# Moving the first sums of squares and the high and low parts of the gate's input in an attention and MoE kernel

## What is computed

```python
attn = softmax(mask(scale * q @ k.T)); x = attn @ v          # x: 1536 rows, 512 columns
rms = np.sqrt(np.mean(x * x, axis=-1, keepdims=True) + 1e-06)
xn = x / rms * rms_g
g = xn @ w_gate
silu = g * (1.0 / (1.0 + np.exp(-g)))
val = xn @ w_val
return (silu * val @ w_out).astype(np.float32)
```

## Time and profile before

| | before |
|---|---|
| median of 3 runs | 808.73 us (807.5 to 809.12) |
| the profiled execution | 808.62 us, span 806.8 us |
| TensorE busy | 778.0 us |
| VectorE busy | 501.6 us |
| ScalarE busy | 374.6 us |
| GpSimd busy | 317.8 us |

### The profile page before, as it was taken

How to read it: one execution, slowest core, us unless ns; L and a number is a source line. 1 busy time by engine, 2 the same in 40 slices (tenths; PEclk the granted TensorE clock), 3 DMA queues, 4 the chain that set the end, 5 groups by cost and what they waited for, 6 DMA issues and landing times.

```text
span 806.8 us, 14337 instructions
## 1 busy us (share of the span) xinstructions
PE 778.0 (96%) x4306; PEld 689.1 (85%) x4306; DVE 501.6 (62%) x979; ACT 374.6 (46%) x668; POOL 317.8 (39%) x340
## 2 busy tenths in 40 slices
PE   7899999999989999999999999999889999999995
PEld 5789888988878999999999988888778887777884
DVE  7999999999984554434343434363674556655640
ACT  5888888888983311111101234434433425553331
POOL 7877777788886363234422002211100111010110
PEclk9999999999997999999999999999999999999999
DMA  7888769656300222111210030031543476455410
GB/s 197 236 233 217 209 165 273 182 140 159 83 2 28 91 68 65 39 39 39 65 52 0 2 155 27 26 133 35 187 157 131 140 247 230 148 199 191 140 51 22
DMA packets 53717, 96.84 MB, mean 120 GB/s; under 512 B 6841, under 2 KB 21189, under 8 KB 53656
## 3 DMA queue, kind: packets, MB, share of 16 engines
q1 hardware_dynamic: 48648, 84.90, 35.7%
q10 hardware_dynamic: 2768, 4.87, 2.3%
q0 software_dynamic: 2240, 6.31, 2.0%
HBM read 58.51 MB, written 21.04 MB: 99 GB/s over the span
## 4 chain that ended last, share of the span: by engine, by line
PE 83%; DVE 8%; issue 3%; POOL 2%; ACT 2%; DMA 1%; ACTq 0%; POOLq 0%; DVEq 0%
PE ps_t L1052 13%; PE ps_s L920 12%; PE ps_t L1122 11%; PE ps_s L1102 11%; PE ps_t L920 6%; PE ps_t L872 6%; DVE pT_l L1470 3%; PE ps_o L920 3%; PE ps_p L920 3%; PE ps_s L859 2%; PE ps_s L858 2%; DVE negmax L1452 2%; PE ps_s L1113 2%; PE ps_o L887 1%; PE ps_o L889 1%
## 5 line engine op out<-in xcount | busy, mean ns | idle before, releaser
L693 POOL TENSOR_SCALAR probs<-probs,rden,alone 128x768 f32<-128x768 f32 x96 | 94.5, 997 | 35.1 <-DVE rden L1464 34.9
L1470 DVE TENSOR_TENSOR pT_l<-ps_t,pT_h 128x384 fp32r<-128x384 f32 x192 | 97.7, 549 | 16.1 <-ACT pT_h L1212 15.0
L801 POOL DMA_INDIRECT out_dram<-rows_out,rows_in x16 | 23.0, 1440 | 194.0 <-ACT rows_out L1367 185.1
L920 PE MATMUL ps_s<-xn,w_h 128*128 128x384 f32 x384 | 98.8, 338 | 0.2 <-POOL w_l L713 0.2
L1212 ACT ACTIVATE pT_h<-ps_t 128x384 fp32r<-128x384 f32 x192 | 85.4, 491 | 25.6 <-PE ps_t L872 24.5
L1202 ACT ACTIVATE probs<-ps_s,negmax 128x768 f32<-128x768 f32 x96 | 87.0, 907 | 19.2 <-DVE negmax L1452 18.7
L872 PE MATMUL ps_t<-ident,probs 128*128 128x128 f32 x576 | 88.5, 284 | 5.7 <-DVE pT_l L1470 2.7
L1630 DVE TENSOR_TENSOR expert_w<-piece,expert_w 128x2048 f32 (+1 forms) x32 | 72.1, 2288 | 32.3 <-ACT expert_w L1335 26.7
L1452 DVE TENSOR_REDUCE negmax<-ps_s 128x1 f32<-128x770 f32 x96 | 90.8, 947 | 1.7 <-PE ps_s L859 1.1
L872 PEld LDWEIGHTS ps_t<-ident,probs 128*128 128x128 f32 x576 | 63.5, 142 | 25.8 <-DVE pT_l L1470 10.3
L1122 PE MATMUL ps_t<-expert_w,hidT_h 128*128 (+1 forms) x256 | 82.2, 402 | 2.3 <-DVE hidT_l L1785 1.4
(11 more groups left out here) (248 smaller groups left out, 1722.2 us busy)
## 6 DMA issues: line engine op xcount, KB each, us to landing
piece<-in_moe_w_dram SPq DMA_DIRECT2D x32, 1024.0 KB, 6.3
routed<-filler SPq DMA_DIRECT2D x52, 257.0 KB, 4.6
k_a<-qk_h SPq DMA_DIRECT2D x28, 192.0 KB
rows_in<-routed ACTq DMA_DIRECT2D x17, 257.0 KB, 2.7
rawv<-in_v_dram SPq DMA_DIRECT2D x8, 384.0 KB, 6.0
w_raw<-in_moe_w_gate_dram SPq DMA_DIRECT2D x12, 256.0 KB, 3.0
w_raw<-in_moe_w_val_dram SPq DMA_DIRECT2D x12, 256.0 KB, 3.4
wo_raw<-in_moe_w_out_dram SPq DMA_DIRECT2D x12, 256.0 KB, 2.6
```

What stands on the lines that cost most here:

```text
L693: nc.gpsimd.tensor_scalar(pr, pr, rden[:, j:j + 1], alone[:, j:j + 1], ALU.mult, ALU.add).then_inc(norm_done, 1)
L920: mm = nc.tensor.matmul(unit_banks[tg][w][:, 0:G], a_[par][:, w, c, :], xn_at(tg, part, c), start=(n == 0), stop=(n == 3 * C - 1))
L1470: nc.vector.tensor_tensor(pT_l[u % 4][:], ps_t[kt % 2][:, 0:G], pT_h[u % 4][:].bitcast(F32), ALU.subtract).then_inc(low_ready, 1)
```

## The change

In the last pair, ScalarE's high parts of batch 0 are made in eight pieces of 384 columns (steps 1, 2, 4, 5, 7, 8, 10, 11) and not in four of 768 (steps 1, 2, 4, 5). TensorE's sum_squares(0) and (1) move from step 1 of the tail to the ends of steps 7 and 10 of the last pair; the second goes to bank ps_o. VectorE copies each result to rms at the end of its own step 7 or 10 (sums_to_rms), counted by sums_out, for which TensorE waits before it uses the bank again (step 9 of the last pair, step 0 of the tail). The root moves from step 1 to step 0 of the tail and the high parts of batch 1 from steps 0, 2, 3 to 1, 2, 3; invert, turn_rinv and rows_of_factors move from step 2 to step 1. VectorE's low parts for the gate go as 2, 2, 1, 1, 2 in steps 0 to 4 and four after the steps (before: 2, 2, 0, 4, 2 and two). For tg 2 and 3 VectorE adds last_square into the partial sum (add_last), so TensorE has three products for each and not six. In high_of the lines behind the new return are not reached. The lines with the names of the two new semaphores, last_added and sums_out, are left out:

```diff
@@ -226,8 +226,7 @@
         POOL_LOWS = [(0, c) for c in range(C)]
-        DVE_LOWS = ([(1, c) for c in range(C)] + [(2, c) for c in range(C - 1)] + [(3, c) for c in range(C - 1)]
-                    + [(2, C - 1), (3, C - 1)])
+        DVE_LOWS = ([(1, c) for c in range(C)] + [(tg, c) for tg in (2, 3) for c in range(C)])
         addr[0] = x2_offset
@@ -383,18 +382,23 @@
         value_banks = (ps_o, ps_p)
-        sum_places = tuple(ps_p[:, HT * tg:HT * (tg + 1)] for tg in range(TG))
+        sum_places = tuple((ps_p, ps_o, ps_p, ps_p)[tg][:, HT * tg:HT * (tg + 1)] for tg in range(TG))
         SQUARES_01 = 12
+        LATE_LOWS = {0: slice(0, 2), 1: slice(2, 4), 2: slice(4, 5), 3: slice(5, 6), 4: slice(6, 8)}
         EARLY = {0: 2, 1: 6, 2: 2, 3: 2, 4: 2, 5: 2}
         def high_of(tg, c):
+
+            if tg < TG // 2:
+                return C * tg + c + 1
+            return 2 * C + c + (1 if c < C - 1 else tg - 1)
             if tg < TG // 2:
 ...
             return C + c + 1 if c < C - 1 else C + c + tg - 1
-        XNH_DONE = 2 * C + 1
+        XNH_DONE = 3 * C + 1
         first_proj_banks = (ps_o, ps_p, ps_t[0], ps_t[1])
@@ -898,8 +902,7 @@
                     pe.wait_ge(factors_row, 1)
-                    pe.wait_ge(last_squared, tg - TG // 2 + 1)
-                    parts.append(last_square[tg - TG // 2])
+                    pe.wait_ge(last_added, tg - TG // 2 + 1)
                 for t in range(HT):
@@ -949,10 +952,10 @@
                         scores(P, par, j)
-                    if not s and j == 1:
-                        pe.wait_ge(x_done, 4 * LAST_PAIR + 2)
-                        sum_squares(0)
-                        sum_squares(1)
+                    if s and not ahead and j == 9:
+                        pe.wait_ge(sums_out, 1)
+                    if not s and j == 0:
+                        pe.wait_ge(sums_out, 2)
                     if not s and j == 3:
@@ -961,9 +964,13 @@
                         values(Pv, par if j >= LAG + 1 else 1 - par, g, jj)
+                    if s and not ahead and j in (7, 10):
+                        pe.wait_ge(x_done, 4 * LAST_PAIR + (j - 7) // 3)
+                        sum_squares((j - 7) // 3)
                     if not s and j in EARLY:
                         some(EARLY[j], first_units)
-                    if not s and j == 2:
+                    if not s and j == 1:
+                        pe.wait_ge(x_done, 4 * LAST_PAIR + 2)
                         turn_rinv(0)
@@ -1226,7 +1233,12 @@
                 cols = slice(HT * tgs[0], HT * (tgs[-1] + 1))
-                nc.scalar.activation(rms[:, cols], ps_p[:, cols], ACT.Sqrt, bias=eps[:],
+                source = rms
+                if tgs[0] == 0:
+                    act.wait_ge(sums_out, 2)
+                else:
+                    source = ps_p
+                nc.scalar.activation(rms[:, cols], source[:, cols], ACT.Sqrt, bias=eps[:],
                                      scale=1.0 / DM).then_inc(rms_made, len(tgs))
@@ -1250,14 +1262,15 @@
                         half_out(Pv, g)
-                    if s and not ahead and j in (1, 2, 4, 5):
+                    if s and not ahead and j % 3:
                         if j == 1:
 ...
                             act.wait_ge(scores_ready, PAIR_STEPS * LAST_PAIR)
-                        high_xn(0, (1, 2, 4, 5).index(j))
-                    if not s and j in (0, 2, 3):
-                        high_xn(1, (0, 2, 3).index(j))
-                    if not s and j == 1:
+                        tg, c = divmod(2 * (j // 3) + j % 3 - 1, C)
+                        high_xn(0, c, cols_of(tg))
+                    if not s and j in (1, 2, 3):
+                        high_xn(1, j - 1)
+                    if not s and j == 0:
                         root((0, 1))
@@ -1482,6 +1495,16 @@
                 nc.vector.reciprocal(rinv[:, cols], rms[:, cols]).then_inc(rinv_made, len(tgs))
+            def sums_to_rms(tg):
+                dve.wait_ge(summed, tg + 1)
+                nc.vector.tensor_copy(rms[:, HT * tg:HT * (tg + 1)], sum_places[tg]).then_inc(sums_out, 1)
+
+            def add_last(half):
+                dve.wait_ge(last_squared, half + 1)
+                dve.wait_ge(square_step, (17, 22)[half])
+                part = sums[TG // 2 + half][0]
+                nc.vector.tensor_tensor(part[:], part[:], last_square[half][:], ALU.add).then_inc(last_added, 1)
+
             def rows_of_factors(b):
@@ -1500,27 +1523,25 @@
                         denoms(P - 1, 3)
-                    if not s and j == 2:
+                    if not s and j == 1:
                         invert((0, 1))
 ...
                         dve.wait_ge(gates_in, 48)
-                    if not s and j < 2:
-                        lows_xn(DVE_LOWS[2 * j:2 * j + 2])
-                    if not s and j == 3:
-                        lows_xn(DVE_LOWS[4:8])
-                    if not s and j == 4:
-                        lows_xn(DVE_LOWS[8:10])
                     Pv, g, jj = steps_of(P, j, LAG + 2)
 ...
                         x_out(Pv, g)
-                    if not s and j == 2:
+                    if s and not ahead and j in (7, 10):
+                        sums_to_rms((j - 7) // 3)
+                    if not s and j == 1:
                         rows_of_factors(0)
+                    if not s and j in LATE_LOWS:
+                        lows_xn(DVE_LOWS[LATE_LOWS[j]])
                     if isinstance(P, int) and P == 0 and j in (1, 2, 3, 4):
@@ -1590,7 +1611,10 @@
             period(8, 0, s=False, ahead=False)
-            lows_xn(DVE_LOWS[10:12])
+            add_last(0)
+            lows_xn(DVE_LOWS[8:11])
+            add_last(1)
+            lows_xn(DVE_LOWS[11:12])
             invert((2, 3))
```

More of the change, by code:

```diff
@@ L276, in build @@
                  "half_ready x_done pool_passed sp_passed "
-                 "consts_made gates_in filled fill_done square_step last_squared summed rms_made rinv_made rinv_turned factors_row factors_out "
+                 "consts_made gates_in filled fill_done square_step last_squared last_added summed sums_out rms_made rinv_made rinv_turned factors_row factors_out "
                  "gained u_made xnh_made xnl_pool xnl_dve w_split wo_split gate_made value_made sig_made silu_step hs_high hs_low y_made x2_made "
@@ L287, in build @@
          half_ready, x_done, pool_passed, sp_passed,
-         consts_made, gates_in, filled, fill_done, square_step, last_squared, summed, rms_made, rinv_made, rinv_turned, factors_row, factors_out,
+         consts_made, gates_in, filled, fill_done, square_step, last_squared, last_added, summed, sums_out, rms_made, rinv_made, rinv_turned, factors_row, factors_out,
          gained, u_made, xnh_made, xnl_pool, xnl_dve, w_split, wo_split, gate_made, value_made, sig_made, silu_step, hs_high, hs_low, y_made, x2_made,
```

## The result

| | before | after |
|---|---|---|
| median | 808.82 us (807.5 to 809.12, 4 runs) | 802.82 us (802.27 to 803.83, 4 runs) |
| the profiled execution | 808.62 us, span 806.8 us | 803.83 us, span 801.9 us |
| TensorE busy | 778.0 us | 772.8 us |
| VectorE busy | 501.6 us | 504.0 us |

The change makes the kernel faster: the ratio is 0.993, with a 95% interval of 0.9913 to 0.9948. The prediction was 798.1 us with a range of 795.6 to 802.6. The sign is right. The time misses the range by 0.2 us and the forecast by 4.7, since the gain is 6.0 us where 10.6 were forecast.

A forecast was written before the change was run, and what follows sets the result against it. TensorE, busy 96% of the span, was taken as the bound. The tail was to save 12.2 - 0.8 = 11.4 us and the last pair to lose 0.9: 808.62 - 11.4 + 0.9 = 798.1 us, range 795.6 to 802.6.

The forecast's parts named there:

- the last pair: Stage before the tail: shorter high parts gain, added sums and copies cost; 0.9 us lost in all.
- the groups named under what would show it: Sign of being right: last-pair groups of three steps taking about 7.5, 7.7 and 7.8 us.
- (a): Tail, step 1: TensorE's wait for x_out ahead of the first sums goes, 1.64 us saved.
- (b): Tail, step 1: the first sums of squares leave this stage, 4.87 us saved.
- (c): Tail: the slow clock behind the first sums goes, 2.8 us saved.
- (d): End of the tail: the last sums halve because VectorE adds last_square first, 1.3 us saved.
- (e): End of the tail: the second slow-clock stretch, behind the last sums, goes, 1.6 us saved.
- the clock falls behind the new pieces: Rival, last pair steps 7 and 10: sums lower the clock, 1.6 us per fall, 801.3 us for two; chance 15%.
- the long slow stretch that would have made the kernel slower: Rival: clock falls at step 7 and stays low until the gate's groups, 12.6 us lost, 810.7 us; chance 4%.
- the step behind the last x_out: End of the tail: VectorE's adds and three lows take 2.75 us, of which 0.1 to 0.3 us shows.
- VectorE becomes the bound: Rival: slow gate lows in steps 1 to 4 cost 2.4 us, dear last pair 2.6; 800.6 or 803.1; chance 13%.

The follow-up runs named there:

- e5: e1 with the first sums of squares, root, inverse, turn_rinv and rows_of_factors back at their places of before; 804.98 us, ratio 0.9966.
- e12: The kernel before, with GpSimd's split_w(1, 1) waiting for VectorE's last gate low; 807.02 us, ratio 0.9986.
- e3: The changed kernel without add_last, so TensorE sums both parts with six products per group; 799.37 us, ratio 0.9906.
- e2: The changed kernel, with GpSimd starting split_w(1, 1) only when VectorE's twelve gate lows are done; 798.75 us, ratio 0.9893.
- e1: The changed kernel, with both add_last ahead of VectorE's four last gate lows; 798.68 us, ratio 0.9892.
- e8: The kernel before, with the first sums moved behind step 1's values and six gate groups in the tail; 803.26 us, ratio 0.9954.
- e9: The kernel before, with the first sums behind step 1's six gate groups and both add_last right behind the last x_out; 808.07 us, ratio 0.9996.
- e11: e9 with GpSimd's split_w(1, 1) waiting for VectorE's last gate low; 803.65 us, ratio 0.9946.
- e6: e1 with ScalarE's high parts of batch 0 whole again, four of 768 columns; 798.03 us, ratio 0.9885.
- e10: The changed kernel with split_w(1, 1) behind VectorE's lows and four whole high parts of 768 columns; 798.88 us, ratio 0.9874.
- e4: The changed kernel, with VectorE's two gate lows ahead of rows_of_factors in step 1 of the tail; 802.78 us, ratio 0.9945.

## Why the prediction was right and where it failed

**Right in the sum: the last pair.** Its forecast was 0.9 us lost. The four groups took 6.71 + 7.47 + 8.22 + 8.31 = 30.71 us against 29.79: 0.92. That is partly luck: steps 0 to 5 won 0.75 us, not 1.3, and steps 6 to 11 lost 1.67, not 2.2. And the groups named under what would show it, 7.5, 7.7 and 7.8 us, do not follow from the sum: with the first at 6.8 they add up to no loss. The last two took 8.22 and 8.31. VectorE idles 0.64 us ahead of its maximum in steps 8 and 11, and a copy to rms took 0.16.

**Right in kind, too large in size: terms (a), (b) and (c).** The tail ran from 241.01 to 260.37 us at a clock of 1.00, with pauses of at most 0.47 us. The pieces of sums, 1.23 us each, brought no fall in the last pair, nor in any experiment that has them; neither "the clock falls behind the new pieces" nor the long slow stretch that would have made the kernel slower came. e5 prices the move at 6.3 us by the medians (3.4 in the profiled executions), where a, b and c were 1.64 + 4.87 + 2.8 = 9.3, and 8.4 with the 0.9 lost in the last pair. In e5 the pause is 1.22, the sums take 2.84 and the slow stretch behind them 3.4 us, of which half is lost. What went wrong is that (b) and (c) hang on how long a slow stretch lasts, and that was read from one execution. The first fall lasted some 10 us there, 3.4 in e5 and 3.4 in e12, whose steady stretch comes 3.2 us earlier from the turn than the kernel before's with the same work on TensorE.

**Failed: the step behind the last x_out.** The prediction said "0.55 + 1.65 + 0.55 = 2.75 us after the last x_out", which TensorE was to cover but for 0.1 to 0.3 us. The 1.65 was taken from lows with GpSimd idle, "since the squares are done by then". The squares were done; the splitting of the next weights was not begun, and the prediction itself says, further on in the same paragraph, that it is released by the same x_done. It asked only whether the splitting would be ready in time, not what it would do to VectorE meanwhile. The three lows took 4.54 us, the pause was 3.09 and the slow clock behind it another 3.2. The bound for a low, "1.35 at the longest", came from a low beside a shorter GpSimd instruction, the squares of 1.01 us; beside w_h of 1.41 and w_l of 2.52 us the lows took 1.40 and 2.69. The kernel before had the warning: its last two lows took 1.94 us beside w_h, and its w_l is 2.53 us long.

```profile
266.98 1.94 DVE L1492 SCALAR_TENSOR_TENSOR xn<-xT,gain,xn 128x384 fp32r<-128x384 f32 x2
...
267.04 1.47 POOL L710 TENSOR_SCALAR w_h<-w_raw 128x1024 fp32r<-128x1024 f32 x1 [10.80 <-DVE xT L1476]
268.60 2.53 POOL L713 TENSOR_TENSOR w_l<-w_raw,w_h 128x1024 fp32r<-128x1024 f32 x1
```

The rival "VectorE becomes the bound" had the mechanism and not the place: it looked at steps 1 to 4 and at 2.4 us. The Trainium skill (SBUF — State Buffer, "Who interferes with whom") has an exclusive lock between a VectorE instruction with two SBUF inputs and a GpSimd one that reads SBUF, the later one waiting for the other whole. The traces agree: three lows in 4.54 us beside 1.41 + 2.52 us of splitting, 1.67 without it. Priced so, at the whole length of the GpSimd instructions, the overlap could have been read from the splitting's rows of before.

**Terms (d) and (e).** (d), 1.3 us, is 1.0 in the traces where the collision is gone (e3 against e2) and 0.3 where it is not (e3 against e1), because TensorE then waits for rinv. The prediction had no wait for rinv behind the lows; in e1 it is 0.85 us. (e), 1.6 us, was not there in each order or execution: with full-length last sums the fall came in the profiled executions of before, e8 and e12, and not in e3's.

## What to carry to other kernels

When a queue is reordered, ask for each new member not only what it waits for and how long it takes alone, but which instructions of other engines are released by the same event, and whether they share a resource with what stands ahead of it; a collision that nobody waited for costs nothing until something needed is put behind it. Where two orders are possible, put what the bounding engine needs next first, and check that what is pushed back is not needed as well (e1 gains 4.1 us by it and still pays 0.85 for rinv, e9 loses 4.8). Where the collision can be put off whole, as in e2, nothing has to be chosen. In this kernel the first sums cost less behind real work than behind a pause (e8, 4.2 us). And a term read from a stretch of slow clock needs more than one profiled execution.

## What the runs showed of the hardware

In these executions a pause and then short products brought the clock down more surely than either alone. Behind a pause of 1.2 to 1.6 us, some 2.6 us of one-column products (at full clock) had a fall with them or right behind them in all three cases: the kernel before, e5 and e12 (first sums). Right behind other work, the same products kept the clock at 1.00 in four cases (e3, and the first sums of e8, e9 and e11) and were followed by a fall in three (second sums of before, e8 and e12). Pauses of 0.85 to 1.46 us with other work behind them (e1, e6, e8, e11), or with 0.80 us of such products (e10), had no fall. Pauses of over 3 us had one in all three cases, at their end or within 1 us behind them (the changed kernel, e4, e9). What decides between the cases was not found.

In the tail, as far as windows of 2 us can tell, a stretch at 0.50 lasted some 3.4 us in six cases (second sums of before and e8, both sums of e12, e4, e5), 6.8 in two (the changed kernel, e9) and 10 in one (first sums of before), though TensorE was busy nearly throughout. e4 and the changed kernel had the same pause of 3.09 us ahead of it, and half the length.

The slow clock goes with the spread from run to run. e12's spans are 802.8 to 803.5 us where the mean granted clock is 0.992, and 805.8 to 807.9 where it is 0.984. At which stage the clock was lost in these executions is not shown, since one execution of each kernel is profiled. The kernels with falls in the tail spread more (5.2 us in e12, 3.6 in e8) than those without (1.7 in e1, 2.4 in e2), but the former were mostly run 11 or 12 times and the latter 4 to 6, so that comparison proves little.
